# Token mixing with z stationary and its result transposed, no turns of u, and three changes of order

## The reference, cut to what matters

```python
# attention: B=4, H=8, S=768, D=64; every key within 128 before the query, and keys 0 to 3
x = attention(q, k, v)                    # (B, S, C), C = H*D = 512
# token mixing
theta = x @ w_theta                       # per token
zr, zi = x * cos(theta), x * sin(theta)
u = x + einsum('ts,bsd->btd', w_tok_r, zr) + einsum('ts,bsd->btd', w_tok_i, zi)
# channel mixing
m = u + maximum(u @ w_ch, 0)
gate = sigmoid(sum_k conv_w[k] * shift(m, 4 - k))   # 5 taps along the tokens
out = (gate * (m @ w_val)) @ w_out        # (B, S, C)
```

## Time and profile before

| | |
|---|---|
| median of 3 runs | 739.53 us (739.35 to 739.87) |
| the profiled execution | 740.86 us, its span 739.1 us |
| TensorE busy | 682.3 us, 92% |
| VectorE, ScalarE, GpSimd busy | 410.1, 294.3, 257.9 us |
| granted TensorE clock, mean | 0.97 |
| attention | about 7 to 200 us of the span |
| token mixing | about 204.6 to 497 us |
| channel mixing | about 499.6 to 739.1 us |

### The profile page before, as it was taken

One profiled execution on the slowest core, in us unless ns is written; L12 is line 12 of the kernel. 1 busy time (PEld: TensorE's weight loads), 2 busy tenths in 40 slices (PEclk: granted clock), 3 DMA queues, 4 the chain that ended last, 5 costly groups with the idle time before them and its releaser, 6 DMA issues. The chain is left out here.

```text
span 739.1 us, 13828 instructions
## 1 busy us (share of the span) xinstructions
PE 682.3 (92%) x3904; PEld 592.5 (80%) x3904; DVE 410.1 (55%) x988; ACT 294.3 (40%) x767; POOL 257.9 (35%) x331
## 2 busy tenths in 40 slices
PE   3999999999747999999999999978399999999997
PEld 2888888888636888888888888867399999999995
DVE  2676666766526446555564465630936745754770
ACT  3666656666314133232231313313344335435332
POOL 3635444453203221221222212303762364355222
PEclk9999999999969999999999999996789999999999
DMA  5555646456230000700150042063102102200111
GB/s 178 163 155 185 189 157 216 143 194 182 69 104 30 29 15 1 227 28 0 51 177 27 0 156 86 15 213 144 43 1 87 54 35 82 85 28 15 43 43 43
DMA packets 43841, 68.25 MB, mean 92 GB/s; under 512 B 3744, under 2 KB 20128, under 8 KB 43680
## 3 DMA queue, kind: packets, MB, share of 16 engines
q1 hardware_dynamic: 43808, 67.85, 28.2%
HBM read 48.97 MB, written 18.87 MB: 92 GB/s over the span
## 5 line engine op out<-in xcount | busy, mean ns | idle before, releaser
L852 POOL TENSOR_TENSOR z_lo<-z_raw,z_hi 128x512 fp32r<-128x512 f32 x48 | 61.4, 1301 | 212.8 <-ACT z_hi L886 212.8
L277 ACT ACTIVATE probs<-masked,neg_max 128x260 f32<-128x260 f32 (+1 forms) x192 | 92.4, 482 | 67.1 <-DVE neg_max L326 65.9
L1015 PE MATMUL acc<-z_hi,w2h 128*128 128x512 f32 x288 | 114.3, 397 | 0.0
L1015 PE MATMUL acc<-z_lo,w2h 128*128 128x512 f32 x288 | 112.3, 390 | 0.0
L1015 PE MATMUL acc<-z_hi,w2l 128*128 128x512 f32 x288 | 112.2, 390 | 0.0
L326 DVE CUSTOM_DVE_ANT_0 masked<-ps_s,mask 128x260 f32<-128x260 f32 (+1 forms) x192 | 69.5, 403 | 57.1 <-PE ps_s L401 52.8
L1292 DVE SCALAR_TENSOR_TENSOR taps<-m_raw,conv_w,taps 128x384 f32<-128x384 f32 x128 | 76.2, 668 | 0.0
L918 DVE TENSOR_TENSOR xT_lo<-ps_x,xT_hi 128x512 fp32r<-128x512 f32 x24 | 16.6, 691 | 98.6 <-ACT xT_hi L873 98.6
L1183 POOL TENSOR_TENSOR g_lo<-g_raw,g_hi 128x384 fp32r<-128x384 f32 x32 | 32.5, 1014 | 101.7 <-ACT g_hi L1230 101.6
L443 PE MATMUL ps_o<-v_sb,probsT 128*128 128x64 f32 x384 | 66.5, 268 | 0.0
L401 PE MATMUL ps_s<-k_sb,q_sb 64*128 64x260 f32 (+1 forms) x384 | 53.4, 398 | 11.2 <-POOL mask L214 11.2
(11 more groups left out here) (94 smaller groups left out, 1518.6 us busy)
## 6 DMA issues: line engine op xcount, KB each, us to landing
k_sb<-kT SPq DMA_DIRECT2D x16, 396.0 KB, 5.3
q_sb<-qT SPq DMA_DIRECT2D x16, 384.0 KB, 4.8
v_sb<-vP SPq DMA_DIRECT2D x16, 384.0 KB, 3.3
x_scratch<-x_sb SPq DMA_DIRECT2D x16, 384.0 KB, 4.2
x_nat<-x_scratch SPq DMA_DIRECT2D x24, 256.0 KB, 3.6
x_res<-x_scratch SPq DMA_DIRECT2D x24, 256.0 KB, 4.1
u_scratch<-u_sb SPq DMA_DIRECT2D x24, 256.0 KB, 2.8
u_nat<-u_scratch SPq DMA_DIRECT2D x8, 768.0 KB, 4.6
```

The source lines that it names most:

```text
L277: nc.scalar.activation(probs[e][:, i, lo:hi], masked[2 * t + e][:, lo:hi], ACT.Exp, bias=neg_max[:, s, e, i:i + 1], scale=-1.0, accum_out= ...
L852: nc.gpsimd.tensor_tensor(z_lo[s % ZR][:, part, :], z_raw[:, part, :], z_hi[s % ZR][:, part, :].bitcast(F32), ALU.subtract).then_inc(z_lo_ ...
L1015: last = nc.tensor.matmul(acc[t][:], l, r, start=s == 0 and m == 0 and a == 0, stop=s == T - 1 and m == 1 and a == 2)
```

## The change

**Attention.** VectorE copies the sinks before the pair's other bank and before `invert`; ScalarE copies them between the exponentials of the first and the second tile of visit 1.

**Token mixing.** `tokens` makes the transposed result. A 128x128 block of z is stationary and the weights stream. `acc[0]` to `acc[3]` hold the four channel blocks for tokens 0 to 511; `acc[4]` and `acc[5]` hold two channel blocks each for the 256 tokens left. ScalarE also copies `ps_x` unsplit (`xT_raw`), SP stores it to `xT_scratch`, and `x_res` is loaded from there; u goes to `uT_scratch`, channels by tokens.

**Channel mixing.** `uT` is loaded as it is; the turns, the bank `ps_t` and both copies out of it are gone, and ScalarE casts `uT_hi` from `uT` (`hi_u`), now behind `hi_m` of the next unit. GpSimd's body is `lo_g(n)`, `lo_m(n+1)`, `lo_u(n+2)`. `ps_c` has four banks.

```diff
@@ attention, ScalarE @@
                         for t in range(2):
                             for e in range(2):
                                 exp(n, s, v, t, e)
+                            if t == 0 and v == 1 and not (first and s == 0):
+                                evac_sinks(n - 1)
                         if not (first and s == 0 and v == 0):
                             evac(k - 1, (v - 1) % VISITS)
-                        if v == 1 and not (first and s == 0):
-                            evac_sinks(n - 1)
@@ attention, VectorE @@
                         if v == 1 and not (first and s == 0):
-                            invert(n - 1, 1 - s)
+                            evac_sinks(n - 1)
                         if not (first and s == 0 and v == 0):
                             evac(k - 1, (v - 1) % VISITS)
                         if v == 1 and not (first and s == 0):
-                            evac_sinks(n - 1)
+                            invert(n - 1, 1 - s)
@@ token mixing, SP @@
+            def load_res(b, j):
+
+                if j < RR:
+                    for t in range(T):
+                        sp.wait_ge(xT_out[t], 16 * (b + 1))
+                        sp.sem_inc(sp_gate2, 1)
+                sp.wait_ge(u_done, T * (b + 1) + j - RR + 1)
                 sp.sem_inc(sp_gate2, 1)
+                sp.dma_start(two_halves(x_res[j % RR], j), bank_of(xT_scr, b, j)).then_inc(res_in[j % RR], 16)
+
+            def store_xT(b, s):
+                sp.wait_ge(xT_raw_done, T * b + s + 1)
+                sp.sem_inc(sp_gate2, 1)
+                sp.dma_start(xT_scr[bass.ds(b, 1), :, s * P:(s + 1) * P].rearrange("o (k p) t -> p (o k) t", p=P),
+                             xT_raw[s % XR][:]).then_inc(xT_out[s], 16)
@@ token mixing, ScalarE @@
                 act.wait_ge(turned2, n + 1)
+                wait_count(act, xT_out[(s - XR) % T], 16 * (b + 1) if s >= XR else 16 * b)
+                nc.scalar.copy(xT_raw[s % XR][:], ps_x[:]).then_inc(xT_raw_done, 1)
                 wait_count(act, theta_done, n - XR + 1)
                 nc.scalar.copy(xT_hi[s % XR][:], ps_x[:]).then_inc(xT_hi_done, 1)
@@ token mixing, TensorE @@
+            def block_of(s, k, bank, cols, first):
+
+                for m in range(2):
+                    at = ((1 - m) * T + s) * S
+                    w = (w2h[:, at + cols.start:at + cols.stop], w2l[:, at + cols.start:at + cols.stop])
+                    z = (z_hi[s % ZR][:, m, k * P:(k + 1) * P], z_lo[s % ZR][:, m, k * P:(k + 1) * P])
+                    for a, (l, r) in enumerate(split_passes(z, w)):
+                        last = nc.tensor.matmul(bank, l, r, start=first and s == 0 and m == 0 and a == 0,
+                                                stop=s == T - 1 and m == 1 and a == 2, skip_group_check=True)
+                return last
...
+                for j in range(T):
                     if s == 0:
-                        pe.wait_ge(u_done, T * b + t + 1)
...
+                        pe.wait_ge(u_done, T * b + j + 1)
+                    if j < CB:
+                        last = block_of(s, j, acc[j][:], slice(0, C), True)
+                    else:
+                        for h in range(2):
+                            last = block_of(s, 2 * (j - CB) + h, acc[j][:, h * (S - C):(h + 1) * (S - C)],
+                                            slice(C, S), h == 0)
@@ channel mixing, SP @@
-                wait_count(sp, turned, CB * (n - 1))
+                wait_count(sp, m_done, CB * (n - 1))
+                wait_count(sp, uT_lo_done, CB * (n - 1))
@@ channel mixing, GpSimd @@
                     lo_g(b, c)
+                    if (n := ahead(b, c, 1, last)):
+                        lo_m(*n)
                     if (n := ahead(b, c, 2, last)):
                         lo_u(*n)
-                    if (n := ahead(b, c, 1, last)):
-                        lo_m(*n)
@@ channel mixing, ScalarE @@
                         hi_g(b, c, k)
-                        if nxt2:
-                            evac_u(*nxt2, k)
                     if nxt:
                         for k in range(CB):
                             hi_m(*nxt, k)
+                    if nxt2:
+                        for k in range(CB):
+                            hi_u(*nxt2, k)
                     evac_out(b, c)
@@ channel mixing, TensorE @@
                     for k in range(CB):
                         values(b, c, k)
-                        if nxt2:
-                            turn(*nxt2, k)
@@
```

More of the change, by code:

```diff
@@ L723, in mix_tokens @@
         x_res = [sb(f"x_res{r}", [P, C]) for r in range(RR)]
+        xT_raw = [sb(f"xT_raw{r}", [P, CB, P]) for r in range(XR)]
         xT_hi = [sb(f"xT_hi{r}", [P, CB, P], F32R) for r in range(XR)]
@@ L744, in mix_tokens @@
         u_out = [sem(f"u_out{r}") for r in range(RR)]
+        xT_out = [sem(f"xT_out{t}") for t in range(T)]
         w3_in = [sem(f"w3_in{j}") for j in range(4)]
@@ L818, in body @@
                         load_x(b + 1, s - 1)
+                    if s < T - 3:
+                        store_xT(b, s + 3)
+                    elif not last:
+                        store_xT(b + 1, s + 3 - T)
+                    if s == T - 2:
+                        for j in range(RR):
+                            load_res(b, j)
                 if last:
@@ L824, in body @@
                         sp.wait_ge(u_out[r], 16 * T // RR)
[L825 to L828, removed]
+                    sp.dma_start(uT0[:], uT_scr[0, :, 0:S // 2].rearrange("(k p) t -> p k t", p=P)).then_inc(u_in0, 16)
+                for j in range(T):
+                    sp.wait_ge(u_done, T * (b + 1) + j + 1)
                     sp.sem_inc(sp_gate2, 1)
[L830 to L835, removed]
+                    sp.dma_start(bank_of(uT_scr, b, j), two_halves(u_sb[j % RR], j)).then_inc(u_out[j % RR], 16)
+                    if j < T - RR:
+                        load_res(b, j + RR)
                 if not last:
                     load_x(b + 1, T - 1)
+            for t in range(3):
+                store_xT(0, t)
             batches(sp, body)
@@ L965, in body @@
                                                 ALU.subtract).then_inc(w3_lo_done, 1)
[L966 to L971, removed]
+                for j in range(T):
+                    dve.wait_ge(acc_done, T * b + j + 1)
+                    dve.wait_ge(res_in[j % RR], 16 * (T // RR * b + j // RR + 1))
+                    wait_count(dve, u_out[j % RR], 16 * (T // RR * b + j // RR))
+                    nc.vector.tensor_tensor(u_sb[j % RR][:], acc[j][:], x_res[j % RR][:],
                                             ALU.add).then_inc(u_done, 1)
@@ L1002, in theta @@
                 last.then_inc(theta_done, 1)
+            def block_of(s, k, bank, cols, first):
[7 more added lines that the diff above has]
+                return last
             def tokens(b, s):
-                n = T * b + s
-                pe.wait_ge(z_lo_done, 2 * n + 2)
-                for t in range(T):
+                pe.wait_ge(z_lo_done, 2 * (T * b + s) + 2)
+                for j in range(T):
                     if s == 0:
-                        pe.wait_ge(u_done, T * b + t + 1)
[L1010 to L1016, removed]
+                        pe.wait_ge(u_done, T * b + j + 1)
+                    if j < CB:
+                        last = block_of(s, j, acc[j][:], slice(0, C), True)
[3 more added lines that the diff above has]
+                                            slice(C, S), h == 0)
                     if s == T - 1:
                         last.then_inc(acc_done, 1)
-                    elif t == T - 1:
+                    elif j == T - 1:
                         last.then_inc(tok_done, 1)
@@ L1063, in mix_channels @@
         w_lo = w3l + [sb("w3_lo2", [P, CB, C], F32R)]
-        u_nat = [u_nat0, sb("u_nat1", [P, UT, C])]
-        uT = [sb(f"uT{r}", [P, CB, L]) for r in range(2)]
+        uT = [uT0, sb("uT1", [P, CB, L])]
         uT_hi = [sb(f"uT_hi{r}", [P, CB, L], F32R) for r in range(2)]
@@ L1135, in _, with body @@
             sp.dma_start(conv_w[:], conv).then_inc(conv_in, 16)
-            load_u(1, 0)
-            def body(b, loads):
+            def body(b, last):
                 for c in range(2):
-                    if c < loads:
-                        load_u(b + 1 + c, 1 - c)
+                    if not last:
+                        load_u(b + 1, c)
                     for j in range(UT):
@@ L1148, in body @@
                                      o_sb[j][:]).then_inc(o_out[j], 16)
[L1150 to L1153, removed]
+            batches(sp, body)
             for j in range(UT):
@@ L1253, in _ @@
             for k in range(CB):
-                evac_u(0, 0, k)
+                hi_u(0, 0, k)
             for k in range(CB):
-                evac_u(0, 1, k)
+                hi_u(0, 1, k)
+            for k in range(CB):
                 hi_m(0, 0, k)
@@ L1318, in _ @@
         def _(pe):
```

(12 more changed lines are left out.)

58 lines of the change are left out of this document (27 added, 31 removed).

## The result

| | before | after |
|---|---|---|
| median | 739.44 us, 6 runs (738.84 to 740.29) | 748.94 us, 6 runs (747.08 to 751.53) |
| ratio of after to before | | 1.0129, 95% interval 1.0107 to 1.0151 |
| profiled execution, span | 740.86 us, 739.1 | 750.17 us, 748.2 |

The account below looks back on a forecast made before the run. The prediction took TensorE, busy 92% of the span, as the bound. Its terms, −7.3 + 1.2 + 4.1 − 3.6 + 8.8 = +3.2 us, on a median of 739.53 gave 742.7 us, range 734 to 750.

Parts of the forecast that it names:

- Attention: Attention's sink matmuls: both waits for the sink copies vanish over 14 pairs, −7.3 us.
- a wait would take the old one's place: Rival in attention: late masks or exponentials return up to 7.3 us, giving 743 to 749.6; chance 0.08.
- Token mixing, the head: Start of token mixing: two unsplit copies of `ps_x` lie on TensorE's way, +1.2 us, between 0.6 and 1.8.
- Token mixing, the matmuls: Token mixing's steps: 12 more matmuls each, with 256 columns taking 0.1205 us, +4.1 us.
- The dearer matmul: Rival in token mixing: 256-column matmuls cost more, 789 us, or 766 with uncovered loads; chance 0.05.
- Channel mixing, the head: Start of channel mixing: `uT` is there already, turns vanish, the clock returns sooner, −3.6 us, range −2 to −5.
- Channel mixing, units 1 to 6: Channel mixing's units: four uT subtractions slow VectorE's taps by 3.0 us a unit, TensorE waits for `g_raw`, +8.8 us.
- the margin: Channel mixing's units: `g_raw` ends 0.4 us before TensorE comes to block 2 of values.
- TensorE idles 2.6 in each. The last unit and the tail keep their time: Channel mixing: TensorE waits 2.6 us in each of six units; the last unit and the tail add nothing.
- The clock falls in the new gaps: Rival in channel mixing: TensorE's idle gaps lower its clock, 1.7 us each, one to four giving 744 to 749; chance 0.15.
- The uT splits are hidden: Rival in channel mixing: GpSimd's uT splits barely slow the convolution, 726.9 us; chance 0.17, wholly or in part.

Follow-up runs that it names:

- a1: The kernel before with only the changed order of the sink copies in attention; 732.39 us, ratio 0.9896 to the kernel before.
- a6: The kernel before, with token mixing's fp32r matmuls for z tiles from the fifth on cut from 512 columns into two of 256; 744.59 us, ratio 1.0059.
- a2: The changed kernel with ScalarE's casts and GpSimd's splits of uT put ahead of those of m in channel mixing; 727.45 us, ratio 0.9824 to before.
- a5: The changed kernel with only two of the four uT splits made in full from unit 2 on, the others over 4 columns; 736.28 us, ratio 0.9945 to before.
- a4: The changed kernel with 12 useless matmuls added ahead of values' third block in units 0 to 6; 744.6 us, ratio 1.0059 to the kernel before.
- a3: The changed kernel, its order kept, with each uT split cut to 4 of 384 columns from unit 2 on; 728.4 us, ratio 0.984 to before.
- a7: The variant with u's splits first, plus splits of u and weight rounding ahead of m's first split in channel mixing's head; 721.11 us, ratio 0.9735 to before.

## Why the prediction was right in part, and wrong in size

- **Attention** (−7.3): right, −7.8 in the changed kernel and −7.2 alone (a1). The rival that a wait would take the old one's place is refuted: the sinks have no idle row.
- **Token mixing, the head** (+1.2): +0.6 in these two traces. TensorE's wait for the second angle chain grew from 3.97 to 4.43, a little less than one copy. Over all nine traces the stretch from the last sink to the first `acc` is 31.7 to 32.2 without the copies (before, a1, a6) and 32.6 to 33.4 with them. On the mean that is +1.0, so the two traces don't tell one copy from two.
- **Token mixing, the matmuls** (+4.1): +4.4, and shown by a6 to come from the number of matmuls: 0.0155 us for each added one. The stores of `xT_raw` and the new way of `x_res`, which the forecast had at nothing, cost nothing: a6, without them, took 267.18 in this stretch and the changed kernel 267.13. The loads are hidden behind 256 columns too. The Trainium skill, "TensorE: Matmul & The Clock Gate", section "LDWEIGHTS (loading the stationary operand)", gives P/1.2 ns for a load, an estimate of 0.107 us for 128 columns, and in Part 3, "The mechanism", lets it overlap only matmuls of other rows of the array. By that rule, the trace and the 0.0155 of a6 do not agree. The dearer matmul, as a rival, is refuted.
- **Channel mixing, the head** (−3.6): −4.2. The first channels block began 1.5 sooner after the stage before (9.21 against 10.73), where the forecast had 1.3, and 2.7 more came by the end of channels(1), where it had 2.3. The stretch from the last `acc` to the first outputs also varies from execution to execution: it is 56.7 to 57.8 in before, a1 and a6, and 53.3 to 55.0 in the changed kernel and a2 to a5. On the mean that is −3.4.
- **Channel mixing, units 1 to 6** (+8.8): the mechanism was right, in its place (`uT_lo` under the taps), its price (3.04 against 3.0, a2 and a5), its waiter (`ps_v` for `g_raw`) and its period without a fall (27.61 and 27.82, against 27.6). It measured +14.6. Of this +10.1 is the period without a fall (3 x 27.61 + 3 x 27.82 = 166.3 against 156.2), 1.3 more than the term because the margin was 0.2 (a5) where the forecast had 0.4, and +4.5 are the three falls.
- **The step that failed** is "TensorE idles 2.6 in each. The last unit and the tail keep their time": the idle time was right (2.55), but the sum counted each gap of TensorE at its length only, and the tail at nothing. Three falls of the clock behind such gaps cost 1.3 to 1.6 each, and one in the tail cost 1.6, together 6.1 of the 9.1 us in the profiled execution.
- **What is left** is +3.0 against the forecast's +3.2. That it agrees so well is in part luck: the 1.3 too little in the units and the 0.3 in the matmuls are made up for by 0.5 in attention and 0.6 in each of the two heads.
- **The clock falls in the new gaps** (0.15, 744 to 749): this rival had the mechanism, 1.7 a fall and the place of three of the falls, and the median lay at its upper end. The fourth came in the tail, behind the very gap (2.31 idle) that the prediction gave as one which the clock outlasts. 0.15 was too little. It was one chance for the whole program, where the changed kernel has seven such gaps in each execution, each with its own chance. By an estimate, with one in three falling an execution without any would be rare (0.06). The six executions took 747.08 to 751.53 and the seven of a4 744.16 to 746.64, which fits falls in all six; only the profiled one's were seen, and the mean clocks (0.963 to 0.970, a4's 0.970 to 0.975) don't settle it.
- **The uT splits are hidden** (0.17, 726.9): refuted as a statement on the changed kernel. But a2 and a3 measured what it would have been worth: 727.45 and 728.4.

The sum of what was measured, −7.8 + 0.6 + 4.4 − 4.2 + 14.6 + 1.5 = +9.1, is the difference of the two spans. Two slips in the prediction's arithmetic change nothing: 5.18/4 is 1.295 and not 1.28, and the upper end for a new wait in attention is 750.0 and not 749.6.

What stays open is why the clock falls behind one gap of 2.65 to 3.0 and not behind the next of the same length.

## What to carry to other kernels

When a subtraction or copy of GpSimd is moved, look first at what VectorE does in the new place: here one exchange of order on GpSimd and on ScalarE, which changed no amount of work, was worth 21 us, three times what the removed turns of TensorE could give in the steady part (1.4 us in each of five units). Price a new gap of TensorE twice, once at its length and once with the fall of the clock behind it, and count the chance for each gap; filling it with useless matmuls (a4) is a quick experiment that separates the two, if you check in the trace which falls it could have reached. A part that gains alone (attention, a1) can be hidden in a change that loses, so try the parts apart: attention's order, the absent turns and u's splits first make 727.45, and the same care in the head makes 721.11.

## What the runs showed of the hardware that I had not expected

- The clock's fall is not a function of the gap's length alone, as far as these traces tell: between two starts of TensorE 2.65 apart, at the same place of the program, it stayed up in the kernel before, in a1, a2, a4, a5, a6 and a7, and it fell in the changed kernel and in a3. The five falls in units and tail (four in the changed kernel, one in a3) came 2.3 to 4.4 us after the last matmul ahead of the gap began, when TensorE was at work again or about to be, and lasted 3.4 us each.
- A tap with one SBUF tensor (`TENSOR_SCALAR`, L1319) is slowed beside GpSimd like one with two: in the chain above it starts 1.1 after the one ahead while `uT_lo` or `m_lo` runs, and 0.33 when nothing does.
- Cutting a 512-column fp32r matmul in two costs 0.0155 us (a6), little more than the 0.013 that each has beyond its columns by the earlier trace rows. Hardly any further charge shows down to 256 columns.
